# A chain of linear attention, gated convolution and expert layers on one core: the transposes of the next block's inputs moved between the two halves of the current block's inner rows

## What is computed

```python
# 1 linear attention, 8 heads of 64
state = gamma * state + k[t] outer v[t];  y[t] = scale * q[t] @ state
# 2 gated convolution layer (512 -> 1024 -> 512)
h = relu(x @ w_in); c = conv3(h, conv_w); x2 = (h * sigmoid(c)) @ w_out
# 3 experts (8 of them, 512 -> 1024 -> 512); e is chosen for each token
e = argmax(x2 @ w_gate), or the token before it keeps its expert (local gate)
out = p[e] * (relu(x2 @ w1[e]) @ w2[e])
```

## Time and profile before

| | |
|---|---|
| median of 3 runs | 420.58 us (420.52 to 420.86) |
| the profiled execution, its own time | 420.84 us |
| its span, first to last instruction | 419.0 us |
| TensorE busy | 407.2 us, 97% of the span |
| mean granted TensorE clock | 0.997 of full speed |
| busy: VectorE, ScalarE, GpSimd | 240.2, 198.6, 97.7 us |

### The profile page before, as it was taken

How to read it: one execution, slowest core, us unless ns; L and a number is a source line. 1 busy time by engine, 2 the same in 40 slices (tenths; PEclk the granted TensorE clock), 3 DMA queues, 4 the chain that set the end, 5 groups by cost and what they waited for, 6 DMA issues and landing times.

```text
span 419.0 us, 7067 instructions
## 1 busy us (share of the span) xinstructions
PE 407.2 (97%) x2597; PEld 342.8 (82%) x2598; DVE 240.2 (57%) x310; ACT 198.6 (47%) x276; POOL 97.7 (23%) x104
## 2 busy tenths in 40 slices
PE   8999999999999999999999999999989999999992
PEld 4888799887889987879778888888878888888881
DVE  4888749982004978677395721226882356675540
ACT  2334678670115765461665522225852445556530
POOL 3354782000000000027603122212222221212220
PEclk9999999999999999999999999999999999999998
DMA  8999900000520009554459292110298304716101
GB/s 299 406 411 419 380 1 2 0 2 0 201 101 0 2 0 367 235 203 161 171 210 404 93 394 95 35 40 28 77 381 337 149 17 150 325 52 242 34 16 25
DMA packets 16153, 67.75 MB, mean 162 GB/s; under 512 B 2623, under 2 KB 4159, under 8 KB 11776
## 3 DMA queue, kind: packets, MB, share of 16 engines
q1 hardware_dynamic: 12928, 58.87, 35.9%
q0 software_dynamic: 2912, 8.13, 5.8%
q10 hardware_dynamic: 288, 0.41, 0.3%
HBM read 58.49 MB, written 10.22 MB: 164 GB/s over the span
## 4 chain that ended last, share of the span: by engine, by line
PE 93%; ACT 1%; issue 1%; DMA 1%; DVE 1%; ACTq 0%; DVEq 0%; POOL 0%; POOLq 0%
PE ps L966 25%; PE ps L968 25%; PE ps L967 24%; PE ps L1232 3%; PE ps L996 3%; PE ps L1017 3%; PE ps L1014 2%; PE ps L1206 2%; PE ps L980 1%; PE ps L1063 1%; DMA kv<-qkv 1%; ACT wx L575 1%; PE ps L1042 0%; PE ps L1138 0%; DVE os L907 0%
## 5 line engine op out<-in xcount | busy, mean ns | idle before, releaser
L887 DVE TENSOR_TENSOR wx<-raw_w,wx 128x1024 fp32r<-128x1024 f32 x56 | 64.7, 1219 | 2.8 <-ACT wx L575 2.8
L900 DVE TENSOR_TENSOR hT<-ps,hT 128x512 fp32r<-128x512 f32 x34 | 23.5, 690 | 60.7 <-ACT hT L634 60.7
L966 PE MATMUL ps<-wx,hT 128*128 128x512 f32 x136 | 56.2, 413 | 2.1 <-DVE hT L900 1.1
L623 ACT ACTIVATE hs<-ps 128x512 f32<-128x512 f32 x34 | 20.3, 597 | 73.8 <-PE ps L968 73.7
L966 PE MATMUL ps<-wx,xT 128*128 128x512 f32 x136 | 54.7, 402 | 0.2 <-DVE xT L922 0.2
L575 ACT CAST wx<-raw_w 128x1024 fp32r<-128x1024 f32 x56 | 54.5, 1050 | 0.0
L968 PE MATMUL ps<-wx,hT 128*128 128x512 f32 x136 | 53.2, 391 | 0.0
L968 PE MATMUL ps<-wx,xT 128*128 128x512 f32 x136 | 53.1, 391 | 0.0
L967 PE MATMUL ps<-wx,hT 128*128 128x512 f32 x136 | 53.0, 390 | 0.0
L967 PE MATMUL ps<-wx,xT 128*128 128x512 f32 x136 | 53.0, 389 | 0.0
L966 PE MATMUL ps<-x,win 128*128 128x384 f32 x128 | 43.2, 337 | 0.0
(11 more groups left out here) (160 smaller groups left out, 732.1 us busy)
## 6 DMA issues: line engine op xcount, KB each, us to landing
raw_w<-w_exp SPq DMA_DIRECT2D x28, 1024.0 KB, 7.6
qk<-qkv SPq DMA_DIRECT2D x7, 768.0 KB, 9.7
raw_first<-w_exp SPq DMA_DIRECT2D x4, 1024.0 KB, 7.9
kv<-qkv SPq DMA_DIRECT2D x4, 768.0 KB, 11.4
x_rows<-x2n SPq DMA_DIRECT2D x11, 256.0 KB, 2.7
kv<-qkv SPq DMA_DIRECT2D x7, 384.0 KB, 9.7
x_early<-x2n SPq DMA_DIRECT2D x10, 256.0 KB, 2.3
win_raw<-w_in SPq DMA_DIRECT2D x4, 512.0 KB, 12.1
```

The costliest lines, as they stand in the source:

```text
L623: nc.scalar.activation(hs[:, 512 * a:512 * a + 512], psP1[:, 512 * a:512 * a + 512], ACT.Relu).then_inc(h_done, 1)
L887: nc.vector.tensor_tensor(wx[:, slot, 1, c], raw, wx[:, slot, 0, c].bitcast(F32), ALU.subtract).then_inc(w2_lo_dve if w else w1_lo_dve, 1)
L900: nc.vector.tensor_tensor(lo, psHT[:, 512 * a:512 * a + 512], hi.bitcast(F32), ALU.subtract).then_inc(hT_done, 1)
L966: mm(o, lh, rl, start=first, stop=False)
```

## The change

`turn_x(g + 1)` is called directly behind `turn_h(g, 0)` instead of behind `w1_part(1, 3)`. Nothing else is touched; block 0 and the order on the other engines stay.

```diff
@@ -1274,9 +1274,9 @@
                 w1_part(1, 0, slot)
                 w1_part(1, 1, slot)
                 turn_h(g, 0)
+                turn_x(g + 1)
                 w1_part(1, 2, slot)
                 w1_part(1, 3, slot)
-                turn_x(g + 1)
                 second_layer(g, e, slot)
```

## The result

The changed kernel takes **423.52 us** (median of 6 runs, 423.37 to 423.68) against 420.77 us for the kernel before beside it (6 runs, 420.52 to 421.06). The ratio is 1.0066 with a 95% interval of 1.0053 to 1.0079: 2.75 us slower, where 3.0 us was forecast. The profiled execution took 423.68 us, its span is 421.9 us.

A forecast was written before the change was run, and what follows sets the result against it. TensorE, busy 97%, was taken to bound the kernel. Lost relu cover, 10 x 0.22 + 4 x 0.19 = 2.96 us, about 3.0, on the 420.58 median gave 423.5 us, range 422.4 to 425.2.

The forecast's parts named there:

- The four transposes cost the same anywhere: `turn_x`'s four transposes on TensorE: 0.44 us in either place, eight in a row 0.88, so their sum changes by nothing.
- The relu is the wait that was uncovered: Before `turn_h(g, 1)`: without `turn_x` in between, ScalarE's relu ends 0.33 us late for the transposes' weight load.
- 0.22 us a block: Loss at `turn_h(g, 1)` in ten blocks: 1.81 us to the second matmul behind the transposes, 1.59 if nothing waited.
- The mark: Second matmul behind `turn_h(g, 1)`'s transposes, in `w2_part(1)`; due 1.81 us after the first layer's last matmul starts, 2.03 before.
- The four blocks that I gave 0.19: Blocks 7, 11, 13, 15: second layer already begins 0.03 us later, so the loss there is 0.19.
- The wait for the first turned half costs nothing of its own: Before `w2_part(0)`: weight load at 268.62, its matmul up to 0.05 us late, swallowed by the relu's wait.
- Blocks 1 and 8 are spared: At their second layer's start TensorE already waits 0.7 and 1.1 us for VectorE; the relu is ready, no loss.
- The gather: `turn_x` waits for it 1.4 us earlier; spare 0.4 us (block 2's rows), 1.1 (block 3's). Late-gather rival: 423.9, chance 0.01.
- No change: Rival: the relu's cover holds at `turn_h(g, 1)`, loss 0 to 0.05 us a block, 420.6 to 421.3; chance 0.05.
- a gain by joined groups: Rival: two transpose groups joined in 16 blocks pay once for entering or leaving, 1.8 us gained, 418.8; chance 0.03.
- a slower hand-over: Rival: TensorE sees the relu 0.25 us after its end, 0.20 more lost in each of 14 blocks, 426.3; chance 0.05.
- a lower clock: Rival: TensorE falls to 1.2 GHz for one block's 48 matmuls, 11 us longer, 434.5 in all; chance 0.01.

The follow-up runs named there:

- The run with no eight in a row: Changed kernel with `turn_x(g + 1)` put between `w1_part(1, 2)` and `w1_part(1, 3)`; 423.58 us against 420.96 for the kernel before, ratio 1.0063.
- the first experiment: Changed kernel with `turn_h(g, 1)` moved behind the first of `w2_part(1)`'s three matmuls, in blocks 1 to 16; 421.13 us against 420.96 for the kernel before, ratio 1.0005.

## Why the prediction was right

- **The four transposes cost the same anywhere.** Right. From the start of `turn_h(g, 0)` to the first layer's last matmul it is 1.58 us before (266.42 to 268.00) and 2.02 now (267.18 to 269.20), 0.44 more. The run with no eight in a row lost as much.
- **The relu is the wait that was uncovered.** Right, and shown three ways: the loss goes when one matmul is put back as cover, it follows a threshold when two or three of the four transposes are moved, and it shrinks with the relu's length. The hand-over was 0.05 us, as in the earlier trace rows. Of the 50 to 100 ns that the Trainium skill has (Advanced Engine Details and Errata, under Network/Comms) that is the lower end.
- **0.22 us a block.** The mark bore out 0.21: from `turn_h(g, 0)` to the mark 3.61 before, 3.82 now. Over a whole block it is 0.19, from 12.28 to 12.47 us between relus of blocks 3 to 6, where 12.50 was named; some 0.02 comes back behind the mark. In block 5 it does so over the next 11 matmuls, which take 2.54 us before (270.03 to 272.57) and 2.52 now (271.00 to 273.52); why is open. In 14 blocks it is 2.7 us where the sum had 2.96, and 2.75 was measured. That the median, 423.52, falls on the 423.5 forecast is in part luck: the loss came 0.2 smaller, and the kernel before ran 0.2 above the 420.58 that the sum started from.
- **The four blocks that I gave 0.19.** (Their second layer starts only 0.01 later in the trace before; the 0.03 is there from its second matmul on.) Up to the mark they do lose less, as forecast: 0.18 (block 11: 3.65 before, 3.83 now) against 0.21. Over the whole block the difference is gone: from `turn_h(11, 0)` to `turn_h(12, 0)` it is 12.30 us before and 12.49 now, 0.19 as in blocks 3 to 6.
- **The wait for the first turned half costs nothing of its own.** Right: the second layer's first matmul starts 0.22 after the last one, at 269.42.
- **Blocks 1 and 8 are spared.** Right. Their waits are 0.6 and 1.1 us, where 0.7 and 1.1 were named.
- **The gather.** No wait in the changed kernel's profile. But my spare time of 1.1 us for block 3's rows came from one execution; in the first experiment the same gather took 1.5 us longer and was waited for. So a late gather was likelier than the 0.01 that I gave it, and cost 0.55 us where it came; 0.4 was named, for the rows of another block.
- **No change, a gain by joined groups, a slower hand-over, a lower clock**: none of these came. The clock kept its full level with eight transposes in a row: the granted clock of the changed kernel from 195 to 420 us is 1.00.

## What to carry to other kernels

An operation that itself waits for nothing can still be worth its place: count what other engines finish while it runs. Before moving it, list every wait that stands behind it in program order, and for each compare when its releaser ends with when the wait is reached without it. A busy share of 97% and a list of waits without an entry don't mean slack: here a relu was early by 0.11 us, and 0.44 us of cover was taken away. And when the weight loads list a wait, its length is not its price; two starts of matmuls on either side of it are.

## What was not expected of the hardware

VectorE's first turned half reached TensorE's weight load after 0.20 to 0.26 us in blocks 2 to 16 of the kernel before, which I took for the hand-over's own length. In the changed kernel it took 0.07 to 0.08 us in nine of these blocks, 0.23 to 0.24 in five (2, 7, 11, 13, 15), and 0.27 in block 8. In the nine, most of the old 0.20 was thus the load's turn behind the transposes and not the semaphore. The run with `turn_x` later bears it out, since there the load has nothing of TensorE's to wait for: 0.07 us in the same nine, 0.23 to 0.24 in the other six. Those six are the first blocks of the experts in the middle, all but the first expert and the last; what makes them longer stays open.

The landing of one and the same gather varied between executions from 7.1 to 8.6 us.
